# Lone queries' mean of the values, moved from a blend on GpSimd into four more rows of the value product

## The reference, cut to what matters

```
mask = q_bucket[:, :, :, None] == k_bucket[:, :, None, :]
scores = scale * np.matmul(q, k.transpose(0, 1, 3, 2))
scores = np.where(mask, scores, -1000000000.0)
scores = scores - np.max(scores, axis=-1, keepdims=True)
attn = np.exp(scores)
attn = attn / (np.sum(attn, axis=-1, keepdims=True) + 1e-09)
return np.matmul(attn, v).astype(np.float32)
```

## Time and profile before

| | us |
|---|---|
| median of 3 runs | 806.08 (805.66 to 809.78) |
| the profiled execution | 804.34 |
| its span | 802.6 |
| PE busy | 755.7 (94% of the span) |
| DVE busy | 439.8 |
| ACT busy | 357.3 |
| POOL busy | 233.1 |

### The profile page before, as it was taken

How to read it: one execution, slowest core, us unless ns; L and a number is a source line. 1 busy time by engine, 2 the same in 40 slices (tenths; PEclk the granted TensorE clock), 3 DMA queues, 4 the chain that set the end, 5 groups by cost and what they waited for, 6 DMA issues and landing times.

```text
span 802.6 us, 11427 instructions
## 1 busy us (share of the span) xinstructions
PE 755.7 (94%) x4141; PEld 622.3 (78%) x4141; DVE 439.8 (55%) x703; ACT 357.3 (45%) x543; POOL 233.1 (29%) x225
## 2 busy tenths in 40 slices
PE   3899999999999995799999999859999999999998
PEld 2677777777777764799999999748888888888886
DVE  4677777877787788456665555533443223222222
ACT  1454556666555553255665555432332323232223
POOL 3158676576767671321211111100000000000000
PEclk9899999999999998699999999979999999999999
DMA  5674444544544302756666765180010100010001
GB/s 124 186 201 100 108 97 116 116 110 103 119 104 104 87 11 56 252 178 221 197 203 224 258 225 190 57 314 5 0 53 1 52 1 1 1 52 1 1 0 53
DMA packets 70163, 85.97 MB, mean 107 GB/s; under 512 B 42223, under 2 KB 44271, under 8 KB 69616
## 3 DMA queue, kind: packets, MB, share of 16 engines
q1 hardware_dynamic: 64784, 74.99, 32.5%
q0 software_dynamic: 2560, 7.34, 2.8%
q10 hardware_dynamic: 2784, 3.18, 1.1%
HBM read 58.76 MB, written 13.63 MB: 90 GB/s over the span
## 4 chain that ended last, share of the span: by engine, by line
PE 85%; ACT 4%; POOL 3%; DMA 3%; issue 2%; DVE 2%; SPq 0%; POOLq 0%; ACTq 0%; DVEq 0%
PE score_ps L1439 11%; PE score_ps L1441 11%; PE score_ps L1440 11%; PE out_pair L1441 7%; PE out_pair L1439 7%; PE out_pair L1440 7%; PE out_pair L1307 4%; PE score_ps L1254 4%; PE out_pair L1309 3%; PE out_pair L1308 3%; ACT probs L727 3%; PE score_ps L1283 3%; PE out_pair L1331 3%; POOL probs_lo L629 2%; PE score_ps L1291 2%
## 5 line engine op out<-in xcount | busy, mean ns | idle before, releaser
L629 POOL TENSOR_TENSOR probs_lo<-probs,probs_hi 128x768 fp32r<-128x768 f32 x60 | 109.1, 1856 | 89.4 <-ACT probs_hi L731 89.4
L1439 PE MATMUL score_ps<-w_hi,h_hi 128*128 128x512 f32 x320 | 126.1, 394 | 0.4 <-DVE h_lo L1203 0.4
L1441 PE MATMUL score_ps<-w_hi,h_lo 128*128 128x512 f32 x320 | 124.7, 390 | 0.0
L1440 PE MATMUL score_ps<-w_lo,h_hi 128*128 128x512 f32 x320 | 124.6, 389 | 0.0
L1196 DVE SCALAR_TENSOR_TENSOR gated<-tclip,out_pair 128x512 f32<-128x512 f32 x48 | 33.1, 689 | 145.2 <-ACT tclip L858 145.2
L1439 PE MATMUL out_pair<-xT_hi,w_hi 128*128 128x512 f32 (+1 forms) x320 | 112.1, 350 | 0.0
L1441 PE MATMUL out_pair<-xT_hi,w_lo 128*128 128x512 f32 (+1 forms) x320 | 110.9, 347 | 0.0
L1440 PE MATMUL out_pair<-xT_lo,w_hi 128*128 128x512 f32 (+1 forms) x320 | 110.9, 347 | 0.0
L858 ACT ACTIVATE tclip<-out_pair,three 128x512 f32<-128x512 f32 x48 | 33.1, 690 | 146.5 <-PE out_pair L1441 146.5
L934 DVE TENSOR_REDUCE rowmax<-score_ps 128x1 f32<-128x768 f32 x96 | 88.7, 952 | 15.8 <-PE score_ps L1254 15.4
L1141 DVE TENSOR_TENSOR w_lo<-w_raw,w_hi 128x1024 fp32r<-128x1024 f32 x72 | 85.9, 1222 | 18.4 <-ACT w_hi L741 18.0
(11 more groups left out here) (182 smaller groups left out, 1302.1 us busy)
## 6 DMA issues: line engine op xcount, KB each, us to landing
w_raw<-in_moe_w SPq DMA_DIRECT2D x32, 1024.0 KB, 9.3
w_raw<-in_moe_w_in SPq DMA_DIRECT2D x4, 1024.0 KB, 7.9
w_raw<-in_moe_w_out SPq DMA_DIRECT2D x4, 1024.0 KB, 12.5
qk_raw<-in_q SPq DMA_DIRECT2D x16, 192.0 KB, 3.8
qk_raw<-in_k SPq DMA_DIRECT2D x16, 192.0 KB, 3.9
v_raw<-in_v SPq DMA_DIRECT2D x16, 192.0 KB, 2.5
k_ext<-q_ext SPq DMA_DIRECT2D x16, 192.0 KB, 2.6
k_pair<-q_ext SPq DMA_DIRECT2D x16, 192.0 KB, 3.1
```

Source lines behind the costliest of these rows:

```text
L629: g.tensor_tensor(probs_lo[:, kc, :], probs[:, kc, :], probs_hi[:, kc, :].bitcast(F32), ALU.subtract).then_inc(lo_done_p, 1)
L1439: mm(out_tile, lhs[0], rhs[0], start=first, stop=False)
L1440: mm(out_tile, lhs[0], rhs[1], start=False, stop=False)
L1441: return mm(out_tile, lhs[1], rhs[0], start=False, stop=last)
```

## The change

The mean no longer has a path of its own behind the value product. PE sums the values of head h over all keys into PSUM with a matrix whose last two columns are ones (`column_sums`, 100 x 65 outputs, plain fp32), DVE splits the sum into a high and a low part on rows 98 and 99 (`keep_mean`), and the value product of head h begins with two more products, of these four rows (96 to 99; the first two are zero) with four rows of `q_ext`: the negated maximum's two parts, which are there already, and two new rows that hold 1 for a lone query and 0 for the others. Since the 65th column holds the count 768, the normalisation that exists divides the sum by it. The flag rows are written by one more instruction in DVE's `minus_max` and turned by the same six products as the maxima (four rows out of `turn_max` in place of two).

Removed: `turn_mean`, the seventh product of `turn_back`, the copies of the mean on ACT and DVE, `find_alone`, `blend_mean` on POOL and all of the last head's separate path. Moved: POOL does `sum_v` ahead of `low_v` rather than behind it; `count(0)` stands behind `turn_back`.

```diff
         k_ext = [at(f"k_ext{i}", [P, S], F32R) for i in range(2)]
-        negmax_hl = at("negmax_hl", [P, C, 2], F32R)
+        negmax_hl = at("negmax_hl", [P, C, 4], F32R)
         x_rows = at("x_rows", [P, C, HEADS, XW], F32)
         out_T = at("out_T", [D + 1, S], F32)
-        mean_T = at("mean_T", [D, P], F32)
...
-        mean_T_ps = out_pair[0:D, 2 * BANK - P:2 * BANK]
-        last_mean_ps = prep_ps[0:D, 0:P]
-        last_back_ps = prep_ps[:, BANK:BANK + XW]
         MEAN = C * (XW + 1)
-        assert MEAN + XW <= BANK and S <= 2 * BANK - P
+        mean_ps = out_pair[0:MR + 4, MEAN:MEAN + D + 1]
+        assert MEAN + D + 1 <= BANK and S + E <= 2 * BANK
         turn_ps = [prep_ps[:, 0:BANK], prep_ps[:, BANK:2 * BANK]]
...
             def store_x(i):
-                sp.wait_ge(x_done, i + 3)
+                sp.wait_ge(x_done, i + 1)
                 sp.dma_start(x_v[i // H, i % H, :, :, :], x_rows[:, :, i, 0:D]).then_inc(x_stored, 16)
...
             first = Head(0, 0)
-            step(g.memset(mean_w[:, :], 1.0 / S))
+            step(g.memset(sum_rows[:, :], 1.0))
+            step(g.affine_select(out=sum_rows[:, :], in_=sum_rows[:, :], compare_op=ALU.is_ge, fill=0.0,
+                                 base=-(MR + 2), pattern=[[1, MR + 4]], channel_multiplier=0))
+            step(g.memset(low_row[:, :], 1.0))
+            step(g.affine_select(out=low_row[:, :], in_=low_row[:, :], compare_op=ALU.is_ge, fill=0.0,
+                                 base=-(MR + 3), pattern=[[0, 1]], channel_multiplier=1))
+            step(g.memset(v_sum[:, :, D:D + 1], float(C)))
             step(g.memset(three[:, :], 3.0))
...
                 if not first and not second:
-                    pool.wait_ge(turned_back, h.i - 1)
+                    pool.wait_ge(mean_full, h.i - 1)
                 g.tensor_tensor(v_three[:, :, :], v_raw[:, h.side, 0:3, :], v_raw[:, h.side, 3:6, :],
                                 ALU.add).then_inc(v_step, 1)
                 pool.wait_ge(v_step, h.i * 2 + 1)
                 g.tensor_tensor(v_two[:, :], v_three[:, 0, :], v_three[:, 1, :], ALU.add).then_inc(v_step, 1)
                 pool.wait_ge(v_step, h.i * 2 + 2)
-                g.tensor_tensor(v_sum[:, h.side, :], v_two[:, :], v_three[:, 2, :], ALU.add).then_inc(v_summed, 1)
-            def blend_mean(h):
-                pool.wait_ge(out_read, h.i + 3)
-                pool.wait_ge(x_done, h.i + 2)
-                g.tensor_tensor(blend[:, :, :], alone[:, h.side, :].unsqueeze(2).to_broadcast([P, C, XW]),
-                                mean_sb[:, h.side, :].unsqueeze(1).to_broadcast([P, C, XW]), ALU.mult).then_inc(b_step, 1)
-                pool.wait_ge(b_step, h.i + 1)
-                rows = x_rows[:, :, h.i, :]
-                g.tensor_tensor(rows, rows, blend[:, :, :], ALU.add).then_inc(x_done, 1)
+                g.tensor_tensor(v_sum[:, h.side, 0:D], v_two[:, :], v_three[:, 2, :], ALU.add).then_inc(v_summed, 1)
...
                         low_probs(h.prev(), kc)
+                sum_v(h, first, second)
                 low_v(h)
-                if not first and not second:
-                    blend_mean(h.prev().prev())
-                sum_v(h, first, second)
...
             first_low(CHUNKS - 1)
-            blend_mean(LAST.prev())
-            pool.wait_ge(mean_kept, 1)
-            pool.wait_ge(f_step, HEADS)
-            pool.wait_ge(x_done, HEADS + 1)
-            g.tensor_tensor(blend[:, :, :], alone[:, LAST.side, :].unsqueeze(2).to_broadcast([P, C, XW]),
-                            mean_sb[:, LAST.side, :].unsqueeze(1).to_broadcast([P, C, XW]), ALU.mult).then_inc(b_step, 1)
...
                 act.wait_ge(prep_full, max_use(h, last) + 1)
-                a.activation(q_ext[h.side][MR:MR + 2, :], prep_ps[0:2, 0:S], ACT.Copy).then_inc(prep_free, 1)
+                a.activation(q_ext[h.side][MR:MR + 4, :], prep_ps[0:4, 0:S], ACT.Copy).then_inc(prep_free, 1)
...
             def copy_out(h):
-                act.wait_ge(mean_turned, h.i + 1)
-                a.activation(out_T[:, :], out_pair[0:D + 1, 0:S], ACT.Copy)
-                a.activation(mean_T[:, :], mean_T_ps, ACT.Copy).then_inc(out_copied, 1)
+                act.wait_ge(pv_done, h.i + 1)
+                a.activation(out_T[:, :], out_pair[0:D + 1, 0:S], ACT.Copy).then_inc(out_copied, 1)
...
-            act.wait_ge(mean_early, 1)
-            a.activation(mean_T[:, :], last_mean_ps, ACT.Copy).then_inc(mean_copied, 1)
-            act.wait_ge(mean_back, 1)
-            act.wait_ge(x_done, HEADS)
-            a.activation(mean_sb[:, LAST.side, :], last_back_ps, ACT.Copy).then_inc(mean_kept, 1)
-            act.wait_ge(pv_done, HEADS)
-            a.activation(out_T[:, :], out_pair[0:D + 1, 0:S], ACT.Copy).then_inc(out_copied, 1)
+            copy_out(LAST)
             gate_exp(1)
...
                 v.tensor_scalar(negmax_hl[:, :, 0], rowmax[:, h.side, :], -MASK / 2, -1.0, ALU.max, ALU.mult).then_inc(m_step, 1)
+                v.tensor_scalar(negmax_hl[:, :, 2:4], rowmax[:, h.side, :].unsqueeze(2).to_broadcast([P, C, 2]), -MASK / 2, None,
+                                ALU.is_lt)
                 dve.wait_ge(m_step, h.i + 1)
                 v.tensor_tensor(negmax_hl[:, :, 1], negmax[:, h.side, :], negmax_hl[:, :, 0].bitcast(F32),
                                 ALU.subtract).then_inc(negmax_ready, 1)
-            def find_alone(h):
-                dve.wait_ge(x_done, h.i + 1)
-                v.tensor_scalar(alone[:, h.side, :], rowmax[:, h.side, :], -MASK / 2, None, ALU.is_lt).then_inc(f_step, 1)
...
                 dve.wait_ge(turned_back, h.i + 1)
-                dve.wait_ge(f_step, h.i + 1)
                 sums = out_ps[0][:, 0:MEAN].rearrange("p (c x) -> p c x", x=XW + 1)
                 v.tensor_scalar(denom[:, h.side, :], sums[:, :, XW], EPS, None, ALU.add).then_inc(n_step, 1)
                 dve.wait_ge(n_step, h.i * 2 + 1)
                 v.reciprocal(recip[:, h.side, :], denom[:, h.side, :]).then_inc(n_step, 1)
                 dve.wait_ge(n_step, h.i * 2 + 2)
                 v.tensor_tensor(x_rows[:, :, h.i, :], sums[:, :, 0:XW],
-                                recip[:, h.side, :].unsqueeze(2).to_broadcast([P, C, XW]), ALU.mult)
-                dve.wait_ge(x_done, h.i + 1)
-                v.tensor_copy(mean_sb[:, h.side, :], out_ps[0][:, MEAN:MEAN + XW]).then_inc(out_read, 1)
+                                recip[:, h.side, :].unsqueeze(2).to_broadcast([P, C, XW]), ALU.mult).then_inc(x_done, 1)
+            def keep_mean(h):
+                dve.wait_ge(mean_full, h.i + 1)
+                rows = slice(MR, MR + 4)
+                v.tensor_scalar(mean_part[rows, :], mean_ps[rows, :], low_row[rows, :], None, ALU.mult).then_inc(mean_step, 1)
+                dve.wait_ge(mean_step, h.i + 1)
+                v.tensor_tensor(mean_k[rows, h.side, :], mean_ps[rows, :], mean_part[rows, :].bitcast(F32),
+                                ALU.subtract).then_inc(out_read, 1)
             def head(h, first=False, second=False, last=False):
                 if not first and not second:
                     normalise(h.prev().prev())
+                if not first:
+                    keep_mean(h.prev())
                 high_v(h)
...
             normalise(LAST.prev())
+            keep_mean(LAST)
             split_probs(LAST, BY_V + 1)
...
             hot_rows(0)
-            dve.wait_ge(x_done, HEADS + 1)
+            dve.wait_ge(x_done, HEADS - 1)
             route(v.tensor_reduce(early_logits[:, :, :], x_rows[:, :, H:HEADS - 1, D:XW].rearrange("p c h e -> p c e h"), AX.X, ALU.add))
-            dve.wait_ge(turned_back, HEADS)
-            sums = out_ps[0][:, 0:MEAN].rearrange("p (c x) -> p c x", x=XW + 1)
-            route(v.tensor_scalar(denom[:, LAST.side, :], sums[:, :, XW], EPS, None, ALU.add))
-            route(v.reciprocal(recip[:, LAST.side, :], denom[:, LAST.side, :]))
-            route(v.tensor_tensor(x_rows[:, :, LAST.i, :], sums[:, :, 0:XW],
-                                  recip[:, LAST.side, :].unsqueeze(2).to_broadcast([P, C, XW]), ALU.mult))
-            dve.wait_ge(b_step, HEADS)
-            v.tensor_tensor(x_rows[:, :, LAST.i, :], x_rows[:, :, LAST.i, :], blend[:, :, :], ALU.add).then_inc(x_done, 1)
+            normalise(LAST)
             pick(1)
...
                 for c in range(C):
-                    last = mm(prep_ps[0:2, c * P:(c + 1) * P], negmax_hl[:, c, :], identr[:, :], start=True, stop=True)
+                    last = mm(prep_ps[0:4, c * P:(c + 1) * P], negmax_hl[:, c, :], identr[:, :], start=True, stop=True)
                 last.then_inc(prep_full, 1)
...
                     pe.wait_ge(v_lo_done, h.i + 1)
-                    pe.wait_ge(out_read, h.i + 2)
+                    pe.wait_ge(out_read, h.i + 3)
+                    for lo, hi in halves:
+                        mm(out_pair[0:D + 1, lo:hi], mean_k[MR:MR + 4, h.side, :], q_ext[h.side][MR:MR + 4, lo:hi],
```

(53 more changed lines are left out.)

## The result

| | before | after |
|---|---|---|
| median, us (before: one run more than the prediction had) | 805.87 (4 runs, 804.57 to 809.78) | 832.19 (4 runs, 831.68 to 833.09) |
| ratio, 95% interval | | 1.0316 [1.0299, 1.0333] |
| the profiled execution, us | 804.34 | 833.09 |
| its span, us | 802.6 | 831.4 |
| mean granted clock of TensorE | 0.977 | 0.959 |

What follows compares the result with a forecast made beforehand. PE's own work and its waits, chiefly at `turn_max`, were taken to bound the kernel. +5.2 + 5.4 + 0.2 - 2.6 = +8.2 us on the profiled 804.34 gave 812.5, as a median 814 us; range 804 to 827.

Steps and rivals of the forecast that it cites:

- What bounds the kernel: Attention heads: PE, busy 94% of the span; its waits, such as at `turn_max`, and its own instructions decide the time.
- `turn_max` behind `v_lo`: Twelve heads: `turn_max` waits for DVE behind `v_lo`, at T (first real score tile) + 15.70; +0.43 each, +5.2 us.
- The mean products: Start of the value product: two added products of 4 rows, 512 and 256 columns, put at 0.35 per head.
- new bound: `column_sums` and `turn_back` wait for ACT's copy of the product, losing 0.13 of PE's gain per head.
- the hope that it slips in ahead of `v_lo`: DVE's first `minus_max` instruction, starting within 0.1 us of `v_lo`, might run first, helping heads 4 to 12.
- Heads 2 and 14 blocked: No branch between `v_lo` and `first_low`, so DVE's last small instruction stands behind `first_low`: 2 x 2.70 = +5.4 us.
- In heads 4 to 12 the branch leaves a gap of 0.12: The five even heads: POOL's gap ahead of `first_low` lets DVE's last small instruction through; no cost beyond 0.43 each.
- That rival: `first_low` blocks DVE's last small instruction in heads 4 to 12 too: 5 x 2.27 = +11.4, 825.5 us; chance 0.27.
- flag instruction stands between: A reason given for heads 4 to 12 being blocked too: the instruction added to DVE's `minus_max`.
- The term that was put at nothing: the clock: PE's waits were priced at their length, 2.70 for a blocked head; the prediction named no clock term or rival.
- the 0.2 of L1325: Head 15: gain of 0.2 from its own removed L1325, counted within the -2.6.
- The tail: Behind head 15: 0.8 + 1.0 + 0.64 = 2.4 us gained, bounds 1.0 and 3.5; -2.6 with L1325.

Runs made afterwards that it cites:

- e1: Changed kernel, with POOL's `first_low` made to wait for DVE's `minus_max` of the head it follows: 804.53 us, 0.9973 of the kernel before.
- e2: Changed kernel, with both POOL's `first_low` and `low_v` made to wait for DVE's `minus_max` of their head: 799.23 us, 0.9906 of the kernel before.
- e3: Changed kernel, with POOL's old order (`low_v` ahead of `sum_v`) and no waits added: 801.97 us, 0.9939 of the kernel before.
- e8: Kernel before, with POOL's `low_v` and all behind it made to wait for DVE's `minus_max` of the head: 823.33 us, ratio 1.0216.
- e9: Changed kernel without the flag instruction in `minus_max`, so a lone query gets 0: 831.62 us, 1.0303 of the kernel before.
- e5: Changed kernel, with idle PE products ahead of the wait for the maxima, 22 in even heads and 3 in odd: 818.60 us, ratio 1.0155.
- e7: Kernel before, with only POOL's `first_low` moved directly behind `low_v` of the even heads, ahead of `blend`: 839.16 us, ratio 1.0406.
- e4: Changed kernel, with idle PE products ahead of the wait for the maxima, 40 in even heads and 6 in odd: 831.57 us, ratio 1.0306.

## Why the prediction was wrong

**What bounds the kernel: right.** PE's own path and its waits decide. Where the long wait at `turn_max` was freed and came back nowhere else (e1, e2, e3), the whole loss went; in e8 it came back at the split probabilities, and the time rose.

**`turn_max` behind `v_lo`: right, but put at over twice its price.** In head 3 of after `turn_max` starts at 82.55, T + 15.74 with T = 66.81 (forecast T + 15.70), but `turn_max` to the next head is 2.21 (205.68 - 203.47), not 2.50: the new product behind `cross` costs 0.15 (205.46 to 205.61 in e2) where I put 0.24, and the twelve products of `turn_back` 1.31 (204.37 to 205.68) where I put 1.39 and 0.12. So an undisturbed head costs +0.18, not +0.43. The mean products erred the other way: e2 reaches `turn_max` at T + 15.27, not at T + 14.92; between the maximum's tile and the first value product they add 0.56 in place of 0.35, and `cross` to `turn_max` takes 0.50 (from 204.20 in e2) in place of 0.35. The "new bound" does not bind: ACT's copy in e2 ends at 205.21 (204.40 + 0.81), before PE comes to `column_sums` at 205.46, so the 0.13 put down for it is nothing. The errors nearly cancel, hence 17.49 against 17.56: the sum is right by luck. The larger mean products also bring DVE later against POOL: its first small instruction starts 0.30 behind `v_lo` (220.37 and 220.07), forecast within 0.1, so the hope that it slips in ahead of `v_lo` was gone.

**Heads 2 and 14 blocked: half right.** Head 14 is (2.62). Head 2 isn't: there POOL runs later against DVE, whose last instruction ends (63.92 + 0.16) before `v_lo` starts. DVE's timeline, then POOL's:

```profile
63.92 0.16 DVE L913 TENSOR_TENSOR negmax_hl<-negmax,negmax_hl 128x6 fp32r<-128x6 f32 x1
```

```profile
64.34 0.94 POOL L608 TENSOR_TENSOR v_lo<-v_raw,v_hi 128x384 fp32r<-128x384 f32 x1
```

**The step that failed: "In heads 4 to 12 the branch leaves a gap of 0.12 ... I take it that these five get through."** The 0.12 was read behind `v_sum`, an instruction of 0.32 us, and it is there again in e3 (0.11). Behind `v_lo`, 0.94 long, the next one starts without a gap at the same branch, in after (220.07 + 0.94 against 220.97) and in e9 (221.22 + 0.94 against 222.12). Why the branch costs nothing there no run tested. All five are blocked, at 20.17 per head where the low clock does not yet reach (T from 84.76 to 104.93): 2.4 more than before, where the forecast had 2.70 for a blocked head. That rival had a chance of 0.27 and the time 825.5. Its "flag instruction stands between" was no reason, as e9 shows.

**The term that was put at nothing: the clock.** I priced a wait of 2.7 at 2.7. In the trace it costs 5 for a pair of heads: odd T to odd T is 40.82 in after (164.86 to 205.68), 37.89 in e5 (`turn_max` to `turn_max`, 180.17 to 218.06), 35.55 before. In the earlier trace rows PE has no pause above 0.2 us, but head 0 of the same trace has one, and it priced the pause. PE's timeline of before:

```profile
27.14 0.52 PE L1268 MATMUL prep_ps<-identr,negmax_hl 128*2 128x128 f32 x6 [2.16 <-DVE negmax_hl L942]
...
28.55 1.65 PE L1291 MATMUL score_ps<-q_ext,k_ext 98*128 98x512 f32 x4 [0.26 <-ACT q_ext L720]
```

Behind a wait of 2.16 `turn_max` still runs at 0.52, the first score tile takes 1.65 in place of 0.97, and the granted clock from 28 to 34 us is 0.50. A forecast of pauses of 2.7 us should have carried this as a rival. Not every such pause costs it: behind the one of 2.61 in e8 (at 249.05) the granted clock is 1.00 up to 258 us. What tells the two apart no run shows.

The clock is also what took the result out of the range. Without it the time would be about 816 us, an estimate: e5's 818.60 less the 2.4 of head 2. That lies near the forecast of 814, and by luck, since five more heads are blocked than forecast while the blocked and the plain heads cost less each.

**The sum.** By the starts T, head 15 begins 29.40 later than before (328.06 against 298.66): six blocked heads at 2.4 are 14.4, seven others (the odd ones from 3 on) at 0.18 are 1.3, heads 1 and 2 nothing, and 13.7 is left. The 15.7 of e5 is the better figure for the clock, since it compares the same heads with the same waits; part of the difference sits in head 15, which took longer in before than the others (18.55 from T to T, 17.77 elsewhere) and would not have done so in after (17.64 from `turn_max` to `turn_max` in e1).

**The tail: right in its sum, not in each term.** From T of head 15 to the experts' first product it is 33.59 before and 31.13 after: -2.46 against the 2.4 forecast for this stretch (the 0.2 of L1325 lies ahead of it). The working behind the 2.4 has a slip: it finds 1.1 for `first_low` and adds 0.8. Up to DVE's split of the third chunk 0.86 is gained (T + 6.40 before, T + 5.54 after), up to `turn_back` 0.66 more (T + 13.91, T + 12.39) where the products were put at 1.0, from there to the logits 0.63 (3.37, 2.74) for the addition put at 0.64; 0.31 behind it was not forecast. PE's timeline of before, then of after:

```profile
298.66 0.97 PE L1291 MATMUL score_ps<-q_ext,k_ext 98*128 98x512 f32 x4
...
332.25 0.58 PE L1439 MATMUL score_ps<-xT_hi,w_hi 128*128 128x256 f32 x1
...
334.93 0.28 PE L1439 MATMUL score_ps<-xT_hi,w_hi 128*128 128x256 f32 x1
```

```profile
328.06 0.96 PE L1257 MATMUL score_ps<-q_ext,k_ext 98*128 98x512 f32 x4
...
359.19 0.58 PE L1394 MATMUL score_ps<-xT_hi,w_hi 128*128 128x256 f32 x1
...
364.24 0.28 PE L1396 MATMUL score_ps<-xT_hi,w_lo 128*128 128x256 f32 x1
```

The experts then take 1.9 longer in this execution. Part of it is the clock again, which comes up 2.7 behind the first product before (334.93) and 5.1 behind it after (364.24); at 0.21 per product in place of 0.12 the 2.4 us more cost about 1.0. The rest I did not follow.

## What to carry to other kernels

A small VectorE instruction on which TensorE waits should not be left to race with a GpSimd instruction that can hold it up: give the GpSimd one a wait for it, if what stands behind it on GpSimd has slack (e2), and look first whether it has (e8). When a step is moved past another, ask which long instruction becomes the neighbour of the small one; a gap read behind a short instruction says nothing of one behind a long one. And a pause of TensorE can cost more than its length: in after about twice, in each of six heads, in e8 once only itself. Look in the trace of the kernel before for one such pause, be it in the first head, before pricing it.

## What the runs showed of the hardware that I had not expected

- A pause of PE of 2.57 us, after which its granted clock was at the low one of its two levels, 1.2 GHz: the granted clock was 0.50 from 224.5 on, the first score tile took 1.63 for four records where it takes 0.94, and 0.94 again in e5, where 22 idle products filled the pause. `turn_max` itself, right behind the pause, still ran at 0.52 as elsewhere; the fall came some 1 us behind the pause in head 10, and over 2 us behind it in head 4, whose next score tile (104.93) follows `turn_max` (102.65) after 2.28, as an undisturbed head's does. The waits of 0.7 and 0.98 in e8 left the clock high (1.00 from 100 to 314 us), and so did its one wait of 2.61: the length of the pause alone does not decide.
- A VectorE instruction on 12 elements per partition stands for the whole of the GpSimd instruction beside it: 2.31 us in place of 0.16. The Trainium skill ("SBUF — State Buffer", section "Who interferes with whom") states that the shared pair of ports is held for the whole instruction and that issue order decides who stands. The rows of after, e3 and e9 agree; those of e7 don't: L939, started at 228.08 and standing behind `w_lo`, stands on behind `blend`, which starts only at 230.25 (3.11 in all), and so in every even head from 2 to 14. What passes at a boundary differs too: in e3 two small ones with a gap of 0.08 (205.64 and 205.72), in after the one that stood and the next without a gap, in e7 none.
- Idle products of 128 columns behind weights of 128 columns cost 0.11 each in a row of 40 (e4); the six of `turn_max`, with weights of 4 columns, cost 0.06 each (223.54 to the next product at 223.89).
- The two mean products, 4 rows deep and 512 and 256 columns wide, cost 0.49 (194.29 to 194.78 in e2), where 768 columns of a score tile, 96 rows deep, cost 0.35 (200.39 to 200.74).
